# Two 64-row matmuls in the two halves of the array for the tail of x_lo, and the last two token blocks unrolled

## The reference, cut to what matters

```
attention-like recurrence over 768 steps, 2 x 8 heads of 40   ->  y
x  = y as 1536 tokens x 320
xn = x / sqrt(mean(x*x) + 1e-6) * rms_g
g  = xn @ w_gate ; val = xn @ w_val            (320 x 1536 each)
x2 = (g * sigmoid(g) * val) @ w_out            (1536 x 320)
out = (sigmoid(x2 @ w_gate2) * (x2 @ w_val2)) @ w_out2
```

## Time and profile before

| | us |
|---|---|
| median of 3 runs | 539.47 |
| lowest and highest | 539.11, 540.45 |
| span of the profiled execution | 536.5 |
| what lies around the span, by the median run | 3.0 |
| TensorE matmuls busy | 503.3 (94%) |
| TensorE weight loads busy | 420.3 (78%) |
| VectorE busy | 263.4 (49%) |
| ScalarE busy | 204.2 (38%) |
| GpSimd busy | 100.5 (19%) |

### The profile page before, as it was taken

How to read it: one execution, slowest core, us unless ns; L and a number is a source line. 1 busy time by engine, 2 the same in 40 slices (tenths; PEclk the granted TensorE clock), 3 DMA queues, 4 the chain that set the end, 5 groups by cost and what they waited for, 6 DMA issues and landing times.

```text
span 536.5 us, 7414 instructions
## 1 busy us (share of the span) xinstructions
PE 503.3 (94%) x2649; PEld 420.3 (78%) x2660; DVE 263.4 (49%) x515; ACT 204.2 (38%) x408; POOL 100.5 (19%) x107
## 2 busy tenths in 40 slices
PE   0988988897999999999999999999999999999996
PEld 0576878897887888888888999888888888888884
DVE  6886489888666455443323565422232222322222
ACT  3444456674554422352223556421222212322122
POOL 3344478686533400000000000000000000000000
PEclk9856599798999999999999999999999999999999
DMA  7655657563534100001012143000001000010001
GB/s 162 190 135 160 162 152 206 155 189 79 154 84 108 58 2 0 1 16 34 24 38 71 32 148 117 1 1 0 0 2 49 1 0 1 0 49 0 0 0 49
DMA packets 18145, 35.33 MB, mean 66 GB/s; under 512 B 2192, under 2 KB 10992, under 8 KB 18112
## 3 DMA queue, kind: packets, MB, share of 16 engines
q1 hardware_dynamic: 17824, 34.38, 23.5%
q10 hardware_dynamic: 288, 0.53, 0.4%
HBM read 31.66 MB, written 2.16 MB: 63 GB/s over the span
## 4 chain that ended last, share of the span: by engine, by line
PE 83%; issue 5%; DVE 4%; POOL 3%; DMA 2%; ACT 2%; SPq 0%; DVEq 0%; ACTq 0%; POOLq 0%
PE bank L1019 49%; PE bank L1034 6%; PE bank L1035 6%; PE bank L1036 6%; PE bank L978 3%; PE bank L1043 3%; PE bank L1042 3%; DMA qk_raw<-qk 2%; PE bank L984 1%; PE bank L967 1%; PE bank L946 1%; PE bank L934 1%; PE bank L1007 1%; PE bank L997 1%; POOL q_st L373 1%
## 5 line engine op out<-in xcount | busy, mean ns | idle before, releaser
L1019 PE MATMUL bank<-x_hi,gv_split 128*128 128x512 f32 (+2 forms) x840 | 253.9, 373 | 0.3 <-ACT hid L499 0.3
L1019 PE MATMUL bank<-x_lo,gv_split 128*128 128x512 f32 (+2 forms) x504 | 183.6, 369 | 0.0
L1019 PEld LDWEIGHTS bank<-x_hi,gv_split 128*128 128x128 f32 x840 | 156.0, 194 | 26.5 <-ACT hid L499 0.5
L802 DVE TENSOR_TENSOR hid<-hid,bank 128x512 f32<-128x512 f32 (+1 forms) x60 | 38.0, 633 | 151.9 <-PE bank L1019 151.7
L1019 PEld LDWEIGHTS bank<-x_lo,gv_split 128*128 128x128 f32 x504 | 98.1, 195 | 15.5
L506 ACT ACTIVATE hid_hi<-hid 128x512 fp32r<-128x512 f32 (+1 forms) x84 | 48.0, 571 | 145.4 <-DVE hid L802 106.1
L499 ACT ACTIVATE hid<-bank 128x512 f32<-128x512 f32 (+1 forms) x84 | 44.6, 531 | 120.4 <-PE bank L1019 120.3
L809 DVE TENSOR_TENSOR hid_lo<-hid,hid_hi 128x512 fp32r<-128x512 f32 (+1 forms) x84 | 54.0, 643 | 42.9 <-ACT hid_hi L506 42.9
L1034 PE MATMUL bank<-hid_hi,wo_split 128*128 128x512 f32 (+1 forms) x168 | 61.4, 365 | 0.3 <-DVE hid_lo L809 0.3
L1035 PE MATMUL bank<-hid_lo,wo_split 128*128 128x512 f32 (+1 forms) x168 | 61.3, 365 | 0.0
L1036 PE MATMUL bank<-hid_hi,wo_split 128*128 128x512 f32 (+1 forms) x168 | 60.6, 361 | 0.0
(11 more groups left out here) (106 smaller groups left out, 499.2 us busy)
## 6 DMA issues: line engine op xcount, KB each, us to landing
qk_raw<-qk SPq DMA_DIRECT2D x24, 480.0 KB, 4.5
gv_raw<-wgv SPq DMA_DIRECT2D x24, 384.0 KB, 3.1
wo_raw<-wo SPq DMA_DIRECT2D x24, 160.0 KB, 2.6
v_sb<-v SPq DMA_DIRECT2D x12, 168.0 KB, 4.4
gate<-og SPq DMA_DIRECT2D x12, 160.0 KB, 4.7
k_sb<-k SPq DMA_DIRECT2D x10, 160.0 KB, 4.4
outT<-y_out SPq DMA_DIRECT2D x6, 256.0 KB, 2.0
s_st<-s_st SPq DMA_DIRECT2D x10, 52.5 KB
```

Source lines behind the costliest of these rows:

```text
L802: ins = nc.vector.tensor_tensor(h, h, v_ps[:, 0:size], ALU.mult)
L1019: mm = pe.matmul(ps[:, 0:size], lhs, rhs, start=(i == 0), stop=(i == len(passes) - 1))
```

## The change

The last pass of the gate, slot 4 against x_lo[:, 2], and that of the value go. In their place a function `tail_rests` runs ahead of both: for the gate partitions 0 to 63 of slot 4 against the same partitions of x_lo[:, 2], for the value partitions 64 to 127. These are two matmuls over 64 rows, one in each half of the array, the first into the gate's bank, the second into the value's, and each starts its bank's sum. The value's slot 4 must for that hold w_hi in partitions 64 to 127 and w_lo in 0 to 63, the other way round than the gate's, so `alpha_w` becomes two columns and w_tail is written by two activations. The product w_lo x_lo of the tail is no longer computed. Since the value's bank is now written at the start of the unit, the wait for `hid_done` stands ahead of the gate passes. And the loop over the last two blocks becomes straight code on the three engines that had it.

```
-        alpha_w = consts[:, C_ALPHA + 2:C_ALPHA + 3]
+        alpha_w = [consts[:, C_ALPHA + 2 + i:C_ALPHA + 3 + i] for i in range(2)]
...
-            with eng.Fori(1, B1 - B0) as n:
+            for n in range(1, B1 - B0):
                 body(n)
...
-                nc.scalar.activation(w_tail[:].bitcast(F32R), gv_raw[n % 2][:, :, 2], ACT.Copy,
-                                     scale=alpha_w).then_inc(gv_rounded, 1)
+                for i in range(2):
+                    ins = nc.scalar.activation(w_tail[:, i].bitcast(F32R), gv_raw[n % 2][:, i, 2], ACT.Copy,
+                                               scale=alpha_w[i])
+                ins.then_inc(gv_rounded, 1)
...
+            def tail_rests(f, start, size):
+
+                cols = columns(start, size)
+                for which, (ps, a, b) in enumerate(((g_ps, 0, R), (v_ps, R, P))):
+                    pe.matmul(ps[:, 0:size], wgv[f][a:b, which, 4], x_lo[a:b, 2, cols], start=True, stop=False)
...
-                          (w[:, 4], x_hi[:, 2, cols]), (w[:, 4], x_lo[:, 2, cols])]
+                          (w[:, 4], x_hi[:, 2, cols])]
                 for i, (lhs, rhs) in enumerate(passes):
-                    mm = pe.matmul(ps[:, 0:size], lhs, rhs, start=(i == 0), stop=(i == len(passes) - 1))
+                    mm = pe.matmul(ps[:, 0:size], lhs, rhs, start=False, stop=(i == len(passes) - 1))
...
+                need(pe, hid_done, u)
+                tail_rests(f, start, size)
                 hidden(g_ps, 0, f, start, size).then_inc(g_done, 1)
             def value_products(u):
                 _, start, size = BLOCKS[u // NF]
-                need(pe, hid_done, u)
                 hidden(v_ps, 1, u % NF, start, size).then_inc(v_done, 1)
...
                     pe.wait_ge(act_done, u)
+                    pe.wait_ge(hid_done, u)
+                    tail_rests(f, n * TB, TB)
                     hidden(g_ps, 0, f, n * TB, TB).then_inc(g_done, 1)
-                    pe.wait_ge(hid_done, u)
                     hidden(v_ps, 1, f, n * TB, TB).then_inc(v_done, 1)
```

## The result

| | us |
|---|---|
| changed kernel, median of 4 runs | 552.07 (549.5 to 554.53) |
| kernel before, median of 4 runs | 539.29 (538.41 to 540.45) |
| ratio | 1.025, 95% interval 1.0203 to 1.0298 |
| span of the profiled execution, after | 547.7 (before 536.5) |

The change costs 12.8 us where 19.6 was forecast. In a second set of runs, on another occasion, the ratio was 1.0235 (1.0181 to 1.029). Rows of the kernel before are named by their group, as in the earlier trace rows. Lines of the new file are 2 to 11 higher: L1007 is now L1009, L1019 (the full passes of hidden) is L1030, L1034 to L1043 are L1045 to L1054, and L1019 is the new pair.

The account below looks back on a forecast made before the run. TensorE's passes times their pace were taken to bound the kernel from about 170 us on. Unit prices of 18.8 us plus a 0.8 us stall, on 539.5, gave 559.1 us; 8-in-10 range 529 to 569.

Parts of the forecast that it names:

- The sign and the mechanism: TensorE, around the 64-row pair: changing the array part drains it and delays weight loads, so slower; chance of slower 0.69.
- The price per unit of 512 columns: TensorE, 60 units: net +0.19 us each, between +0.05 and +0.25, 11.4 us together.
- The lag of the second half: TensorE, within the pair: the second half's load trails the first's by 0 to 0.11 us, taken as 0.05.
- The price of 256 columns: TensorE, 24 units: net +0.31 us each, between +0.17 and +0.37, 7.4 us together.
- "hidden" and "at the lower clock": Attention stage: part of the price vanishes in waits for other engines, a lower clock raises it; taken to cancel.
- The stall on hid_done: Start of block 3: the earlier wait for the value bank stalls once, some 0.8 us; hidden in the steady stage.
- The weights: w_tail by two activations: nothing to 0.49 us more, 24 times; taken as nothing, upper bound 2.4 us.
- The loop: Last two blocks unrolled: nothing gained or lost, 0 with 1 us either way.
- Outside the span: Median of the runs lies 3.0 us above the profiled span, which the change doesn't touch.
- Rival 1: 64-row pair: halves run side by side and changing rows costs no emptying; faster, 529.9 us; chance 0.22.
- Rival 2: 64-row pair: halves don't overlap and the emptying is paid; 32 us slower, 571 us; chance 0.08.
- Rival 3: 64-row pair: no overlap and no emptying, so time unchanged, 539 to 540 us; chance 0.10.

Follow-up runs that it names:

- e2: Changed kernel with the two x_lo tail passes over all 128 rows, everything else kept: 538.54 us, 1.0032 times the kernel before.
- e3: Changed kernel with the two 64-row passes apart, each in front of its own gate or value passes: 599.45 us, 1.111 times the kernel before.
- e6: The changed kernel, unchanged, timed again in the same rounds as the kernel before: 552.03 us, ratio 1.0235.
- e4: Kernel before with only the loop over blocks 5 and 6 unrolled: 537.11 us, 0.9986 times the kernel before.
- e1: Changed kernel with both 64-row passes in the same half of the array, so they can't stream together: 565.17 us, 1.0512 times the kernel before.
- e5: Kernel before, unrolled, with half passes of two units sharing one visit in blocks 2, 4, 5 and 6: 535.26 us, 0.9936 times the kernel before.

## Why the prediction was right, and where its sizes were off

- **The sign and the mechanism.** The step that carried it, that leaving and entering a selection of array rows costs a load that can't run ahead and the emptying of the array, held for 64 rows as it was read from 10 rows and 40 columns. e2 against the changed kernel isolates it (rows alone), e3 shows that it is paid per visit.
- **The price per unit of 512 columns**, +0.19, was +0.16. The two gaps were right to the hundredth (0.32, 0.43). The lag of the second half, taken as 0.05, is nil: the two loads start together. The step from the first full pass to the next is 0.34, where I had 0.32. Together that is 0.03 a unit, 60 x 0.03 = 1.8 us too much.
- **The price of 256 columns**, +0.31, was +0.27 in block 3 (3.12 us against 2.85). Where it stands in the attention stage, 12 units, it isn't seen: both kernels reach unit 24 at the same time in their traces, after 12 such units and 12 of 512 columns. In block 1 the changed kernel does lose 1.5 us (units 12 to 24 take 87.4 us against 85.9), so block 0 gave it back or never paid. Forecast were 12 x 0.31 = 3.7 us for block 0; traces with equal granted clocks put it between -0.9 and +1.4 (e6). I had let "hidden" and "at the lower clock" cancel; that was the larger part of the overestimate, some 3 to 4 us of the 6.8. What hides the price there, such as waits for other engines, stays open.
- **The stall on hid_done** at the start of block 3 was 0.88 us where 0.8 was forecast, and at that place only. But the kernel before waited 0.28 us at the same place for ScalarE, so by the waits it cost 0.6 net. By the lengths of TensorE's units it was 0.4: the three units around it grew from 9.98 us (294.47 to 304.45) to 11.21 (296.36 to 307.57), of which 3 x 0.27 is the price. The term was 0.2 to 0.4 too large.
- **The weights.** Taken as nothing while the longer units cover it, which held (3.12 against the loop of 2.95 in e2). The pair of activations costs 0.18 us more, seen only in e2.
- **The loop**: nothing, as said (e4).
- **Outside the span** I took 3.0 us from the median; the executions with a recorded span lie 1.8 above it (549.5 against 547.7). It cancels in the difference.
- **Rival 1** had the overlap right and the switch wrong: a unit of 5.34 to 5.4 us was not seen. **Rival 2** is what e1 builds: it takes 1.051 times the kernel before, with a unit of 5.97 us and not 5.73. **Rival 3**, no overlap and no emptying, is out: its unit is 5.57 us, e1 shows that the halves overlap and e3 that the change of the array part is paid. The Trainium skill's rule in "TensorEngine Tiling (Array Packing)", Tiling Modes, that a change of tiling mode drains TensorE, agrees with 0.32 and 0.43 us around the pair. The Trainium skill's rule in "TensorE: Matmul & The Clock Gate", Part 3, that matmuls in different row groups start some 4 ns apart, agrees too: a pair is busy for 0.503 us where one matmul is shown as 0.500. Each rule alone gives a wrong sign or size here; the sum needs both.

In one line: a visit costs 0.32 + 0.43 + 0.34 = 1.09 us in which one pair slot and two full passes do work, 3 x 0.232 = 0.70; the 0.39 above it is the price, and it saves as many passes as it holds pairs. One pair: +0.39 - 0.23 = +0.16. Two pairs: +0.39 - 0.46 = -0.07, measured -0.08.

## What to carry to other kernels

Two half-height matmuls side by side do run in the time of one, but a visit to another part of the array had a fixed price here, 0.39 us or 1.7 passes of 512 columns, and over 3 passes of 256. Look for a place where the trace already changes the array part and read start to start and the weight loads around it, and count the pairs per visit before writing the kernel; where one pair doesn't pay, free PSUM banks may let several units share a visit.

## What the runs showed of the hardware that was not expected

- Two weight loads for different row halves start at the same time and cost together what one costs (0.19 us shown, and the same 0.43 us from pair to full pass as for a single 64-row matmul in e3).
- The two gaps are the same for 10 and for 64 rows, 0.32 and 0.43 us, so between these two the number of rows selected makes no difference.
- A second matmul in the same half of 64 rows adds 0.23 us to the visit (0.66 against 0.43 us), which is the plain pace, though the two start 0.34 apart: within a visit there is nothing more to pay. A second pair adds 0.24 (e5).
